# Reordering the last token group of a two-layer fp32 MLP: both inward halves together, outward sums in spare banks, the final half summed batch by batch

## The reference, cut to what matters

```python
def _moe2_ref(x, w_in, w_out):          # x 1536 x 320, w_in 320 x 2048, w_out 2048 x 320
    h = x @ w_in
    sp = np.where(h > 20.0, h, np.log1p(np.exp(np.minimum(h, 20.0))))
    g = h * np.tanh(sp)
    return (g @ w_out).astype(np.float32)
```

## Time and profile before

| | us |
|---|---|
| median of three runs | 455.99 |
| the profiled execution, its own time | 457.6 |
| its span (first to last event of the core) | 455.8 |
| TensorE matmul busy | 440.8 (97%) |
| ScalarE busy | 277.0 (61%) |
| VectorE busy | 265.4 (58%) |
| GpSimd busy | 162.7 (36%) |

### The profile page before, as it was taken

How to read it: one execution, slowest core, us unless ns; L and a number is a source line. 1 busy time by engine, 2 the same in 40 slices (tenths; PEclk the granted TensorE clock), 3 DMA queues, 4 the chain that set the end, 5 groups by cost and what they waited for, 6 DMA issues and landing times.

```text
span 455.8 us, 9575 instructions
## 1 busy us (share of the span) xinstructions
PE 440.8 (97%) x3515; PEld 430.8 (95%) x3515; DVE 265.4 (58%) x550; ACT 277.0 (61%) x476; POOL 162.7 (36%) x131
## 2 busy tenths in 40 slices
PE   6999799999999999999999998999999999999996
PEld 5889798999999999999999998999999999999996
DVE  5453779558576755854624565668545664656450
ACT  4548544723642562462237469898797779777980
POOL 2155343422232142223219604644422452254323
PEclk9569979999999999999999999999999999999999
DMA  6739141015014101910034130000000000000000
GB/s 184 219 108 288 53 149 45 2 49 193 0 47 131 61 1 58 285 33 1 1 91 111 55 113 3 1 2 30 1 30 0 0 29 0 0 29 0 29 1 29
DMA packets 14890, 28.06 MB, mean 62 GB/s; under 512 B 1616, under 2 KB 7504, under 8 KB 14864
## 3 DMA queue, kind: packets, MB, share of 16 engines
q1 hardware_dynamic: 14576, 27.05, 19.7%
q10 hardware_dynamic: 288, 0.66, 0.5%
HBM read 25.71 MB, written 2.00 MB: 61 GB/s over the span
## 4 chain that ended last, share of the span: by engine, by line
PE 75%; ACT 7%; issue 7%; DVE 5%; POOL 3%; DMA 2%; SPq 1%; ACTq 0%; POOLq 0%; DVEq 0%
PE bank L1049 32%; PE bank L1057 30%; PE bank L1017 5%; PE bank L990 3%; POOL act_lo L435 2%; DMA qs<-q_t 2%; PE bank L1002 2%; PE bank L1033 1%; DVE act L782 1%; PE bank L1027 1%; ACT soft L591 1%; ACT soft L594 1%; DVE wi_lo L280 1%; ACT decay L474 1%; ACT wi_hi L270 1%
## 5 line engine op out<-in xcount | busy, mean ns | idle before, releaser
L1049 PE MATMUL bank<-x_lo,wi_hi 128*128 128x256 f32 x576 | 155.2, 284 | 0.0
L1057 PE MATMUL bank<-wo_hi,act_hi 128*128 128x320 f32 x384 | 120.5, 314 | 4.5 <-POOL act_lo L435 3.1
L1057 PE MATMUL bank<-wo_hi,act_lo 128*128 128x320 f32 x384 | 118.7, 309 | 0.0
L1057 PE MATMUL bank<-wo_lo,act_hi 128*128 128x320 f32 x384 | 118.6, 309 | 0.0
L1049 PE MATMUL bank<-x_hi,wi_hi 128*128 128x256 f32 x384 | 111.5, 290 | 0.0
L1049 PEld LDWEIGHTS bank<-x_lo,wi_hi 128*128 128x128 f32 x576 | 110.9, 193 | 0.0
L1049 PE MATMUL bank<-x_hi,wi_lo 128*128 128x256 f32 x384 | 109.0, 284 | 0.0
L213 POOL TENSOR_TENSOR act_lo<-act,act_hi 128x512 fp32r<-128x512 f32 x42 | 55.2, 1315 | 147.4 <-ACT act_hi L501 147.4
L435 POOL TENSOR_TENSOR act_lo<-hid,act_hi 128x512 fp32r<-128x512 f32 x48 | 66.1, 1407 | 100.7 <-ACT act_hi L602 100.7
L1057 PEld LDWEIGHTS bank<-wo_hi,act_hi 128*128 128x128 f32 x384 | 72.4, 188 | 6.2 <-issue 4.2
L1049 PEld LDWEIGHTS bank<-x_hi,wi_hi 128*128 128x128 f32 x384 | 74.1, 193 | 1.1 <-issue 0.3
(11 more groups left out here) (110 smaller groups left out, 600.2 us busy)
## 6 DMA issues: line engine op xcount, KB each, us to landing
stage<-w_out SPq DMA_DIRECT2D x8, 640.0 KB, 5.7
decay<-neg_top_rows SPq DMA_DIRECT2D x8, 512.0 KB, 3.8
stage<-w_in SPq DMA_DIRECT2D x6, 512.0 KB, 7.2
ks<-k_t SPq DMA_DIRECT2D x12, 160.0 KB
qs<-q_t SPq DMA_DIRECT2D x12, 160.0 KB
kt<-k_tok SPq DMA_DIRECT2D x6, 320.0 KB, 5.8
out<-out_sb SPq DMA_DIRECT2D x12, 160.0 KB, 1.8
v<-v_tok SPq DMA_DIRECT2D x5, 328.0 KB, 5.0
```

Of the source, the lines that this page charges most:

```text
L1049: last = pe.matmul(dst, w, x, start=(n == 0), stop=(n == len(parts) - 1))
L1057: last = pe.matmul(acc[b][:, 0:DM], a[:, t], w[:, j, :], start=(first and n == 0), stop=(last_tile and n == 2))
```

## The change

TensorE's and ScalarE's loops over groups end one group earlier, and the rest is written out. TensorE runs inward units 10 and 11 together, then outward units 9, 10 and 11; `keep_warm` is gone. Outward units 10 and 11 sum in `turn2` (banks 2 and 3) in place of `acc`. Unit 11 is summed by `last_unit`: all four pieces for batch 0, then all four for batch 1, with a signal for each batch. ScalarE runs unit 10 and unit 11 one after the other and moves finish(4) behind unit 11's high parts; then it copies each batch's sum as it is signalled. VectorE's last copy is gone. The queue stores each batch on its own signal.

```diff
@@ sync
-        with sp.Fori(0, G) as g:
+        with sp.Fori(0, G - 1) as g:
             store(g)
+        for b in range(NB):
+            sp.wait_ge(last_out[b], 1)
+            sp.dma_start(out[bass.ds((G - 1) * L + b * CH * L, L), :], out_sb[:, b, :]).then_inc(stored, 16)
         sp.wait_ge(stored, 16 * NB * G)
@@ scalar
-        with act_.Fori(1, G - 1) as g:
+        with act_.Fori(1, G - 2) as g:
...
-        exps(2 * G - 1)
-        logs_and_tanhs(2 * G - 1)
-        highs_of(2 * G - 1, 1)
+        exps(2 * G - 3)
+        x2_high(G - 1)
+        logs_and_tanhs(2 * G - 3)
+        highs_of(2 * G - 3, 1)
+        for half in range(2):
+            exps(2 * G - 2 + half)
+            logs_and_tanhs(2 * G - 2 + half)
+            highs_of(2 * G - 2 + half, half)
+        act_.wait_ge(stored, 16 * NB * (G - 2))
+        finish(G - 2)
         act_.wait_ge(stored, 16 * NB * (G - 1))
-        finish(G - 1, 1)
+        for b in range(NB):
+            act_.wait_ge(last_sum[b], 1)
+            act_.activation(out_sb[:, b, :], turn2[b][:, 0:DM], ACT.Copy).then_inc(last_out[b], 1)
@@ vector
         products(2 * G - 1)
-        dve.wait_ge(outs2, PU * 2 * G)
-        dve.wait_ge(stored, 16 * NB * (G - 1))
-        dve.tensor_copy(out_sb[:, 1, :], acc[1][:, 0:DM]).then_inc(final_ready, 1)
@@ tensor
+        def last_unit(j):
+
+            for b in range(NB):
+                for p in range(PU):
+                    pe.wait_ge(low2, PU * j + p + 1)
+                    for t in (2 * (PU + p), 2 * (PU + p) + 1):
+                        last = project_out(act2_hi[:, 1, p, :], act2_lo[:, 1, p, :], t, wo2_hi, wo2_lo, False,
+                                           t == FT - 1, turn2, (b,))
+                last.then_inc(last_sum[b], 1)
...
-        with pe.Fori(1, G - 1) as g:
+        with pe.Fori(1, G - 2) as g:
             in_of(g, 1)
             turn_x2(g + 1)
             out_unit(2 * g, 0, g)
             in_of(g + 1, 0)
             out_unit(2 * g + 1, 1, g)
+        in_of(G - 2, 1)
+        turn_x2(G - 1)
+        out_unit(2 * G - 4, 0, G - 2)
+        in_of(G - 1, 0)
         in_of(G - 1, 1)
-        out_unit(2 * G - 2, 0, G - 1)
-        keep_warm(WARM[3])
-        out_unit(2 * G - 1, 1, G - 1)
+        out_unit(2 * G - 3, 1, G - 2)
+        out_unit(2 * G - 2, 0, G - 1, True, turn2)
+        last_unit(2 * G - 1)
```

More of the change, by code:

```diff
@@ L194, in build @@
     outs2, final_ready, stored = s("outs2"), s("final_ready"), s("stored")
+    last_sum, last_out = [s(f"last_sum{b}") for b in range(NB)], [s(f"last_out{b}") for b in range(NB)]
     y2_ready, y2_turned, y2_high, x2_ready = s("y2_ready"), s("y2_turned"), s("y2_high"), s("x2_ready")
@@ L602, in highs_of, with finish @@
                 act_.activation(act2_hi[:, half, p, :], hid[:, p, :], ACT.Copy).then_inc(high2, 1)
-        def finish(g, batches=NB):
+        def finish(g):
             act_.wait_ge(outs2, PU * 2 * (g + 1))
-            for b in range(batches):
+            for b in range(NB):
                 act_.activation(out_sb[:, b, :], acc[b][:, 0:DM], ACT.Copy).then_inc(final_ready, 1)
@@ L1050, in project_in, with project_out @@
             return last
-        def project_out(hi, lo, j, whi, wlo, first, last_tile):
-            for b in range(NB):
+        def project_out(hi, lo, j, whi, wlo, first, last_tile, dst=acc, batches=range(NB)):
+            for b in batches:
                 t = slice((j % 2) * GT + b * L, (j % 2) * GT + (b + 1) * L)
                 for n, (a, w) in enumerate([(hi, whi), (hi, wlo), (lo, whi)]):
-                    last = pe.matmul(acc[b][:, 0:DM], a[:, t], w[:, j, :], start=(first and n == 0),
+                    last = pe.matmul(dst[b][:, 0:DM], a[:, t], w[:, j, :], start=(first and n == 0),
                                      stop=(last_tile and n == 2))
@@ L1215, in _, with out_unit @@
         steps(G - 1, None, None)
-        def out_unit(j, half, g, first=False):
+        def out_unit(j, half, g, first=False, dst=acc):
             if half == 0 and not first:
@@ L1225, in out_unit @@
                     last = project_out(act2_hi[:, half, p, :], act2_lo[:, half, p, :], t, wo2_hi, wo2_lo, t == 0,
-                                       t == FT - 1)
+                                       t == FT - 1, dst)
                 last.then_inc(outs2, 1)
+        def last_unit(j):
+            for b in range(NB):
+                for p in range(PU):
[4 more added lines that the diff above has]
+                last.then_inc(last_sum[b], 1)
         def in_of(g, half, first=False):
```

## The result

The changed kernel takes 453.58 us, the median of 13 runs (452.08 to 455.27), against 455.99 for the kernel before (13 runs beside them, 454.69 to 458.89): a ratio of 0.9945 with a 95% interval of 0.9925 to 0.9964. That is 2.4 us less (1.6 to 3.4 by the interval); forecast were 1.7 us less, 454.3.

What follows compares the result with a forecast made beforehand. The last unit's chain of waits was taken to bound the end, 3.01 us of waiting on TensorE. Last matmul 1.15 us earlier plus 0.49 behind it make 1.64, taking 455.99 to 454.3 us; range 453.2 to 455.6.

Steps and rivals of the forecast that it cites:

- the order of work: TensorE, units 10 and 11: inward unit 11 runs without waiting, outward unit 10 ends at 442.09 as before, straight-line code costs nothing.
- the chain up to the first exp: ScalarE, unit 11: free at 428.05 to start unit 10's highs, first exp 2.08 us later at 430.13.
- the cost of the batch order: TensorE, last unit: summing all pieces batch after batch costs 1.14 us against the old order.
- The likeliest branch: Whole kernel: last Ln 2.29 us earlier, held by VectorE's clips; 454.3 us, bounds 453.9 to 455.0, chance 0.62.
- the clips: VectorE, unit 11: minima blocked by GpSimd's low parts hold the last Ln to 436.45, losing 1.3 us of ScalarE's gain.
- rival (a): VectorE, unit 11: first minimum gets in before GpSimd's third low part, last clip about 0.7 us earlier; 453.6 us, chance 0.12.
- I move this pattern to T = 428.05: VectorE, unit 11: clips keep unit 10's offsets from the start of the highs, so the last clip ends at 436.36.
- The three waits: TensorE, last unit: 0.88 us of work per low part arriving every 1.26 makes it wait before pieces 1, 2 and 3.
- The wait of 0.72 before the first piece: TensorE, last unit: stands 0.72 us for GpSimd's first low part and starts at 442.81.
- Behind the last matmul: Copy and store at the end: only one DMA issue is left, so it goes out 0.49 us sooner.
- Rival (c): Unit 11's chain doesn't move, first low part still at 444.95; batch order costs 1.14, store gives 0.49: 456.6 us, chance 0.13.
- Rival (d): TensorE, last unit: without the constants the clock falls to 0.50, last 30 matmuls take 4.4 us more: 458.7 us, chance 0.08.

Runs made afterwards that it cites:

- last piece by batch: Changed kernel with pieces 0 to 2 of the last unit summed for both batches, only piece 3 by batch: 452.02 us, ratio 0.9908 to the kernel before.
- inward unit 11 put back: Changed kernel with inward unit 11 again behind outward unit 9: end stretch (first matmul of inward unit 10 to span end) 44.28 us, changed kernel 40.44.
- both batches: Changed kernel with the last unit summing both batches piece by piece throughout: from first matmul of inward unit 10 to span end 39.46 us, changed kernel 40.44.
- sums in acc: Changed kernel with units 10 and 11 summed in acc, finish(4) before unit 11's highs: first matmul of inward unit 10 to span end 47.57 us, against 40.44.
- the later exps: Changed kernel with a 64-column ScalarE copy ahead of unit 11's exps: first matmul of inward unit 10 to span end 41.13 us, against 40.44.

## Why the prediction was right

The time lies in the range, and the order of work, the chain up to the first exp and the cost of the batch order came out as worked out. The likeliest branch (0.62) did not happen: of the steps below, the clips went the way of rival (a), which the range took in. Rival (a) named 453.6, and the median is 453.58; so close a hit is luck, since the profiles show 2.71 us less and the medians 2.41, and since two terms that no rival had, 0.23 us behind the last matmul and 0.07 at the restarts, came on top.

**The order of work** came out as worked out: inward unit 11 without a wait, 15.35 us for both inward units (15.36 forecast), outward unit 10 done at 29.43 after the first matmul of inward unit 10 (29.44 forecast), no cost of the straight-line code.

**ScalarE's chain** did, too: highs of unit 10 at 425.25 (forecast, moved by the 2.79 of the start: 425.26), first exp at 427.33 (427.34). A table load again costs 1.31 in all, from the end of the last Ln (433.50) to the first tanh (434.81).

**The clips** bind, as forecast: the last Ln waits for VectorE. Their size was wrong. The step "I move this pattern to T = 428.05" failed: the first exp came as expected, but VectorE's copy followed the exp's end (427.90) by 0.09, where in unit 10 it had followed by 0.20 (415.81 + 0.57 to 416.58). The minimum was issued at 428.60, before GpSimd's third low part (428.70) rather than behind it, and the last Ln started at 432.87, 0.79 before the forecast 433.66. That is rival (a), for which I gave 0.12; a margin of 0.03 us doesn't bear the 0.62 that I gave the other side.

The trace of the kernel before already had the 0.09, in unit 11 itself: the exp ends at 431.35, the copy starts at 431.44. The pattern that I moved was that of unit 10, whose clips stand in VectorE's loop, while those of unit 11 stand behind it, written out. In the loop VectorE's sequencer runs a register operation between its waits and the copy; the last of them is at 419.4, with unit 10, and unit 11 has none.

```profile
430.76 0.59 ACT L585 ACTIVATE soft<-bank 128x512 f32<-128x512 f32 x1
...
431.44 0.69 DVE L912 COPY hid<-bank 128x512 f32<-128x512 f32 x1 [2.33 <-PE bank L1049]
...
L911 DVEq ALU_OP  x24: 40/40/47, 312.6 to 419.4; - x24
```

No run tried this alone, but it holds in every profile: in all seven that have ScalarE's new order, the minima in place and nothing put ahead of the exps (changed twice, last piece by batch twice, inward unit 11 put back, both batches, sums in acc) the first minimum of unit 11 got in, at 0.42. And where it was made to miss (the later exps), the rest of the forecast came out: last Ln at 23.76 for 436.45 - 412.65 = 23.80, last matmul's end at 38.47 for 38.58.

**The last unit.** The three waits stood where forecast, and the cost of the batch order, 1.14 us, was measured as 1.09 and 1.10 at the last matmul (1.14 and 1.06 by end stretches). The wait of 0.72 before the first piece was not there, since the first low part was early. The end behind the last low part was then 30 matmuls, as worked out: the last matmul ended 37.74 after the first of inward unit 10, against 451.23 - 412.65 = 38.58 forecast; 0.84 less. The low parts, early by what the clips gave, make 0.77 of it (last one done at 441.60 + 1.28 = 442.88, forecast 446.44 - 2.79 = 443.65), and restarts 0.05 behind a low part instead of 0.15 the rest, less 0.03.

**Behind the last matmul** I had 0.49 and it gave 0.72. The second issue's going gave 0.52; in addition the queue issued 0.02 behind the copy (448.08 to 448.10) instead of 0.16, and ScalarE's copy started 0.04 behind the last matmul instead of 0.10, which stays open. The issue is written out now, while it stood in a loop before, and in the loop two register operations stand ahead of each issue (first two rows, of the kernel before); the written-out one has none (last row, of the changed kernel):

```profile
L369 SPq FUSED_REGOPS  x12: 46/46/57, 309.9 to 453.5; - x12
L369 SPq MOVE out<-out_sb x12: 29/29/29, 310.0 to 453.5; - x12
...
L376 SPq DMA_DIRECT2D out<-out_sb x2: 342/342/342, 444.6 to 448.1; - x2
```

That the last copy of acc[1] was VectorE's before is not the reason: it ended with ScalarE's (452.42 + 0.49 = 452.91), and the changed kernel's store of group 4, in the loop and behind copies of ScalarE alone, still goes out 0.18 behind the second (439.31 + 0.42 to 439.91).

The sum: 1.64 forecast, plus 0.84 and 0.23 (0.72 - 0.49), is the 2.71 measured.

**Rival (c)** is out: the chain moved by 3.08. **Rival (d)** did not happen, with starts 0.41 apart, but it is real: in the runs with 2.75 us and 5.29 us of nothing on TensorE the clock fell to 0.50, and that cost 0.85 and 2.7 us.

## What to carry to other kernels

At the end of a pipeline the limit moves from the bound engine to the chain that feeds it, so bring forward the work that starts the chain, and give it the banks to do so. Before splitting the last unit for an earlier store, compare what TensorE gets for each delivery of its feeder with the feeder's time: here 0.88 us of work came for every 1.26, and the split cost 1.1 where 0.1 to 0.2 was to be had; splitting only the last piece takes the one without the other. A pattern read inside a loop can't be moved to the code behind it to a tenth of a us: by the traces, the register operations of the loop fall away there. Compare versions by a stretch that starts behind the part that varies.

## What the runs showed of the hardware that was not expected

A minimum of VectorE that meets a GpSimd instruction costs 0.42, 0.92 or 1.5 us, by when it is issued: it ends 0.28 to 0.29 behind the instruction under way. 0.16 us of delay on another engine made the end 0.69 later.

The granted clock need not fall in the wait: in the version with inward unit 11 put back it was 1.00 through 2.75 us of nothing and for 1.8 us of work after, fell to 0.50 just behind 445, and was back by 449. In the version with sums in acc it fell towards the end of the wait (5.29 us).

Register operations in a loop stand in the path between a signal and what it releases: VectorE's copy started 0.20 behind the exp's end in unit 10, in the loop, and 0.09 behind it in unit 11, written out, in the profile before as in the one after; the queue's issue went out 0.16 to 0.18 behind the copy in the loop and 0.02 behind it written out.

What makes the start of the kernel vary by up to 2.8 us between executions is open. The granted clock differed there, 0.50 from 12 to 30 in the profile before and 1.00 there in the last-piece version, but that version's start was no shorter than that of the changed kernel, where it was 0.50 from 14 to 26.
